# Output weights and Fourier table side by side in one tile, and products with the folded rows regrouped from 194 and 384 columns to 290 and 288

## The reference, cut to what matters

```
state = alpha[:, :, t, :, None] * state + einsum('bhd,bhe->bhde', k[:, :, t], v[:, :, t])
y[:, :, t] = einsum('bhd,bhde->bhe', q[:, :, t], state)          # stage 1: a decaying state

gate_pre = sum over 5 taps of conv_w[k] * x shifted by k         # stage 2
x = (sigmoid(gate_pre) * (x @ w_val)) @ w_out

u = x + real(fft(fft(x, axis=1), axis=2))                        # stage 3
un = (u - mean(u)) / sqrt(var(u) + 1e-06)
out = u + maximum(un @ w_ch1, 0) @ w_ch2
```

## Time and profile before

| | |
|---|---|
| median of 3 runs | 563.99 us |
| profiled execution, its own time | 564.29 us |
| its span | 562.50 us |
| PE, DVE, ACT busy | 551.8, 387.9, 215.4 us |
| granted TensorE clock | 0.995 of full speed |
| batch 1: front part (first "val" to first "h") | 182.06 to 215.53 |
| batch 1: MLP part | 215.53 to 313.49, 97.96 us |
| first "h" of batches 0, 1, 2, 3 | 82.53, 215.53, 346.96, 477.52 |

### The profile page before, as it was taken

One profiled execution on the slowest core, in us unless ns is written; L12 is line 12 of the kernel. 1 busy time (PEld: TensorE's weight loads), 2 busy tenths in 40 slices (PEclk: granted clock), 3 DMA queues, 4 the chain that ended last, 5 costly groups with the idle time before them and its releaser, 6 DMA issues.

```text
span 562.5 us, 13474 instructions
## 1 busy us (share of the span) xinstructions
PE 551.8 (98%) x5631; PEld 530.0 (94%) x5631; DVE 387.9 (69%) x870; ACT 215.4 (38%) x502; POOL 16.1 (3%) x35
## 2 busy tenths in 40 slices
PE   7999999999999999999999999999999999999995
PEld 6988999999999999999999999999999999999995
DVE  8899889978857786877676586877936474542321
ACT  5565455434352235325352135425243134222210
POOL 0010000000000000000000000000000000000000
PEclk8999999999999999999999999999999999999999
DMA  8678111332211010223111001222000000000000
GB/s 261 213 252 312 44 43 32 104 89 61 61 43 45 29 43 19 60 67 95 48 47 41 29 5 40 65 72 89 2 26 5 29 0 2 1 12 18 28 1 29
DMA packets 16235, 34.60 MB, mean 62 GB/s; under 512 B 3312, under 2 KB 6640, under 8 KB 15920
## 3 DMA queue, kind: packets, MB, share of 16 engines
q1 hardware_dynamic: 13632, 27.20, 16.0%
q0 software_dynamic: 2112, 6.29, 3.1%
q10 hardware_dynamic: 432, 0.27, 0.2%
HBM read 29.03 MB, written 4.72 MB: 60 GB/s over the span
## 4 chain that ended last, share of the span: by engine, by line
PE 94%; DVE 2%; DMA 1%; issue 1%; ACT 1%; SPq 0%; POOL 0%; DVEq 0%
PE bank L933 44%; PE bank L1018 27%; PE evens L960 4%; PE bank L1003 4%; PE bank L998 2%; PE bank L1086 2%; PE bank L1049 2%; PE sums L980 2%; PE sums L969 2%; DMA v_in<-in_v_dram 1%; PE bank L1130 1%; PE bank L1120 1%; PE bank L1055 1%; DVE w_lo L866 0%; SPq L489 0%
## 5 line engine op out<-in xcount | busy, mean ns | idle before, releaser
L915 DVE SCALAR_TENSOR_TENSOR h_lo<-bank,h_hi 128x256 fp32r<-128x256 f32 x144 | 60.5, 422 | 108.6 <-ACT h_hi L684 104.1
L933 PE MATMUL bank<-unT_hi,w_hi 128*128 128x256 f32 x432 | 124.6, 288 | 0.3 <-DVE unT_lo L691 0.2
L933 PE MATMUL bank<-unT_lo,w_hi 128*128 128x256 f32 x432 | 122.2, 283 | 0.0
L933 PE MATMUL bank<-unT_hi,w_lo 128*128 128x256 f32 x432 | 121.6, 282 | 0.0
L684 ACT ACTIVATE h_hi<-bank 128x256 fp32r<-128x256 f32 x144 | 54.8, 381 | 163.3 <-PE bank L933 163.2
L1018 PE MATMUL bank<-w_hi,h_hi 128*128 128x384 f32 x288 | 99.9, 347 | 0.0
L1018 PE MATMUL bank<-w_lo,h_hi 128*128 128x384 f32 x288 | 97.7, 339 | 0.0
L1018 PE MATMUL bank<-w_hi,h_lo 128*128 128x384 f32 x288 | 97.3, 338 | 0.0
L933 PEld LDWEIGHTS bank<-unT_hi,w_hi 128*128 128x128 f32 x432 | 81.3, 188 | 3.0 <-DVE h_lo L915 0.9
L933 PEld LDWEIGHTS bank<-unT_hi,w_lo 128*128 128x128 f32 x432 | 81.7, 189 | 0.0
L933 PEld LDWEIGHTS bank<-unT_lo,w_hi 128*128 128x128 f32 x432 | 81.5, 189 | 0.0
(11 more groups left out here) (187 smaller groups left out, 1049.5 us busy)
## 6 DMA issues: line engine op xcount, KB each, us to landing
v_in<-in_v_dram SPq DMA_DIRECT2D x24, 224.0 KB, 2.8
w_raw<-in_w_dram SPq DMA_DIRECT2D x2, 2304.0 KB, 10.7
out_dram<-u POOLq DMA_DIRECT2D x24, 192.0 KB, 2.4
a_in<-in_alpha_dram SPq DMA_DIRECT2D x44, 96.9 KB, 2.2
q_in<-in_q_dram SPq DMA_DIRECT2D x44, 96.0 KB, 2.2
k_in<-in_k_dram SPq DMA_DIRECT2D x44, 96.0 KB, 2.2
dftd<-in_dft_d_dram SPq DMA_DIRECT2D x1, 582.0 KB, 4.5
wval_raw<-in_w_val_dram SPq DMA_DIRECT2D x1, 576.0 KB, 5.2
```

The lines of the kernel that those rows point to most:

```text
L915: dve.scalar_tensor_tensor(h_lo[:, f % HBUF, :], ps[:, 0:GW], 0.0, h_hi[:, f % HBUF, :].bitcast(F32), ALU.max, ALU.subtract).then_inc(s_re ...
L933: last = pe.matmul(ps, l, r, start=(i == 0), stop=(i == len(mms) - 1))
```

## The change

The tiles wd_hi and wd_lo go. The tiles of the output weights become 772 columns wide (MIX): cosines in 0 to 193, the weights in 194 to 577, sines in 578 to 771. A product may now take any run of neighbouring columns:

- "u" takes 290: the cosines and the first 96 columns of z for the sums.
- "zsum" takes the other 288 of z.
- "v" takes 290: the last 96 columns of z for the differences, and the sines. For the first block it takes 386: the last 192 of z and the sines.
- "zdif" takes the first 288 of z for blocks 1 and 2. For the first block it is replaced by "zrow", 386 columns: the cosines and the first 192 of z.

ACT copies the z columns of each product to its place in u. The number of matmuls stays, but for "wdl", which now needs two per block of 194 columns each. All of `w_out` is needed from the first "vpre" on, where it was needed from the first "zdif" on.

```diff
+MIX = 2 * NC + D
+ZU = 96
+ZV = (192, ZU, ZU)
@@ SCHEDULE, front part
-    sch.append(("zdif", b, 0, 0))
+    sch.append(("zrow", b, 0, 0))
@@ tiles
-        WEIGHTS = [("wval", D), ("wout", D), ...
+        WEIGHTS = [("wval", D), ("wout", MIX), ...
-        wd_hi = sb("wd_hi", [128, K, 2 * NC], F32R)
-        wd_lo = sb("wd_lo", [128, K, 2 * NC], F32R)
+        mix_hi, mix_lo = w_hi["wout"], w_lo["wout"]
+        ZCOLS = slice(NC, NC + D)
+        WAVES = (slice(0, NC), slice(NC + D, MIX))
@@ loading w_out
-                            sp.dma_start(w_raw[name][:, :, :], srcs[name]).then_inc(s_wload[WN.index(name)], 16)
+                            dst = w_raw[name][:, :, ZCOLS] if name == "wout" else w_raw[name][:, :, :]
+                            sp.dma_start(dst, srcs[name]).then_inc(s_wload[WN.index(name)], 16)
@@ ACT
                 elif kind == "wd":
-                    act.activation(wd_hi[:, a, :], ps[:, 0:2 * NC], ACT.Copy).then_inc(s_hi, 1)
+                    for i, wave in enumerate(WAVES):
+                        last = act.activation(mix_hi[:, a, wave], ps[:, i * NC:(i + 1) * NC], ACT.Copy)
+                    last.then_inc(s_hi, 1)
                 elif kind == "u":
                     act.wait_ge(s_unit, done(w))
+                    act.activation(u[:, 2 * a + 1, 0:ZU], ps[:, NC:NC + ZU], ACT.Copy)
                     act.activation(U_hi[:, a, :], ps[:, 0:NC], ACT.Copy).then_inc(s_hi, 1)
                 elif kind == "vlo":
                     act.wait_ge(s_unit, done(v_))
                     if a == 0:
-                        act.activation(first_hi[0:1, :], ps[0:1, 0:NC], ACT.Copy)
-                    act.activation(V_hi[:, a, :], ps[:, NC:2 * NC], ACT.Copy).then_inc(s_hi, 1)
+                        wait_for(act, s_out, 16 * STORES * b)
+                    act.activation(u[:, 2 * a + 2, D - ZV[a]:D], ps[:, 0:ZV[a]], ACT.Copy)
+                    act.activation(V_hi[:, a, :], ps[:, ZV[a]:ZV[a] + NC], ACT.Copy).then_inc(s_hi, 1)
+                elif kind == "zrow":
+                    act.wait_ge(s_unit, done(w))
+                    act.activation(u[:, 2, 0:D - ZV[0]], ps[:, NC:NC + D - ZV[0]], ACT.Copy)
+                    act.activation(first_hi[0:1, :], ps[0:1, 0:NC], ACT.Copy).then_inc(s_hi, 1)
                 elif kind in ("zsum", "zdif"):
                     act.wait_ge(s_unit, done(w))
-                    if w[:1] + w[2:] == ("zdif", 0, 0):
-                        wait_for(act, s_out, 16 * STORES * b)
-                    act.activation(u[:, 2 * a + (1 if kind == "zsum" else 2), :], ps[:, 0:D],
-                                   ACT.Copy).then_inc(s_aread, 1)
+                    dst = u[:, 2 * a + 1, ZU:D] if kind == "zsum" else u[:, 2 * a + 2, 0:D - ZV[a]]
+                    act.activation(dst, ps[:, 0:D - ZU], ACT.Copy).then_inc(s_aread, 1)
@@ PE
                 elif kind == "wdl":
-                    pe.matmul(bank[BANK[w]][:, 0:2 * NC], neg[:, :], wd_hi[:, a, :], start=False, stop=True,
-                              skip_group_check=True).then_inc(s_unit, 1)
+                    for i, wave in enumerate(WAVES):
+                        last = pe.matmul(bank[BANK[w]][:, i * NC:(i + 1) * NC], neg[:, :], mix_hi[:, a, wave], start=False,
+                                         stop=True, skip_group_check=True)
+                    last.then_inc(s_unit, 1)
                 elif kind == "u":
-                    product(ps[:, 0:NC], [(sum_hi[:, k_, cols], sum_lo[:, k_, cols], wd_hi[:, k_, 0:NC],
-                                           wd_lo[:, k_, 0:NC]) for k_ in range(K)]).then_inc(s_unit, 1)
+                    product(ps[:, 0:NC + ZU], [(sum_hi[:, k_, cols], sum_lo[:, k_, cols], mix_hi[:, k_, 0:NC + ZU],
+                                                mix_lo[:, k_, 0:NC + ZU]) for k_ in range(K)]).then_inc(s_unit, 1)
                 elif kind in ("vpre", "v"):
-                    n = 0 if a == 0 else NC
+                    here = slice(NC + D - ZV[a], MIX)
...
+                elif kind in ("zsum", "zdif", "zrow"):
+                    here = {"zsum": slice(NC + ZU, NC + D), "zdif": slice(NC, NC + D - ZU),
+                            "zrow": slice(0, NC + D - ZV[0])}[kind]
```

More of the change, by code:

```diff
@@ L193 @@
 assert len(set(SCHEDULE)) == len(SCHEDULE)
-UNIT_KINDS = ("val", "v", "zdif", "u", "zsum", "oddrow", "pq", "pqe", "pqo", "t", "h", "out", "tapj", "wd", "wdl")
+UNIT_KINDS = ("val", "v", "zrow", "zdif", "u", "zsum", "oddrow", "pq", "pqe", "pqo", "t", "h", "out", "tapj", "wd", "wdl")
 def order_of(*kinds):
@@ L203 @@
 UNIT_AT = order_of(*UNIT_KINDS)
-HI_AT = {("v",) + w[1:] if w[0] == "vlo" else w: j for w, j in order_of("u", "vlo", "t", "h", "wd").items()}
+HI_AT = {("v",) + w[1:] if w[0] == "vlo" else w: j for w, j in order_of("u", "vlo", "zrow", "t", "h", "wd").items()}
 ACT_READ = ("zsum", "zdif", "tapj", "wdl")
 AREAD_AT = order_of(*ACT_READ)
-READS = {"pair": "pq", "vlo": "v", "comb": "pqo"}
+READS = {"pair": "pq", "vlo": "v", "zrow": "zrow", "comb": "pqo"}
 DREAD_AT = {(READS.get(w[0], w[0]),) + w[1:]: j
-            for w, j in order_of("val", "u", "vlo", "oddrow", "pair", "comb", "t", "h", "out").items()}
+            for w, j in order_of("val", "u", "vlo", "zrow", "oddrow", "pair", "comb", "t", "h", "out").items()}
 for b_ in range(B):
@@ L217, in bank_plan @@
     front_banks = {("val", 0, 0): 0, ("val", 0, 1): 3, ("val", 1, 0): 1, ("val", 1, 1): 4, ("val", 2, 0): 2, ("val", 2, 1): 0,
-                   ("v", 0, 0): 3, ("v", 1, 0): 1, ("v", 2, 0): 4, ("zdif", 0, 0): 2, ("u", 0, 0): 0, ("u", 1, 0): 3,
+                   ("v", 0, 0): 3, ("v", 1, 0): 1, ("v", 2, 0): 4, ("zrow", 0, 0): 2, ("u", 0, 0): 0, ("u", 1, 0): 3,
                    ("u", 2, 0): 1, ("zsum", 0, 0): 2, ("oddrow", 0, 0): 0, ("pq", 0, 0): 4, ("zdif", 1, 0): 3,
@@ L384, in part @@
                 return t[:, j, :]
+            if WN[i] == "wout":
+                return t[:, :, ZCOLS]
             return t[:, :, :].rearrange("p k n -> p (k n)")
@@ L592, in _ @@
                     act.wait_ge(s_unit, done(w))
-                    act.activation(wd_hi[:, a, :], ps[:, 0:2 * NC], ACT.Copy).then_inc(s_hi, 1)
+                    for i, wave in enumerate(WAVES):
+                        last = act.activation(mix_hi[:, a, wave], ps[:, i * NC:(i + 1) * NC], ACT.Copy)
+                    last.then_inc(s_hi, 1)
                 elif kind == "wdl":
                     act.wait_ge(s_unit, done(w))
-                    act.activation(wd_lo[:, a, :], ps[:, 0:2 * NC], ACT.Copy).then_inc(s_aread, 1)
+                    for i, wave in enumerate(WAVES):
+                        last = act.activation(mix_lo[:, a, wave], ps[:, i * NC:(i + 1) * NC], ACT.Copy)
+                    last.then_inc(s_aread, 1)
                 elif kind == "tapj":
@@ L892, in _ @@
                     dve.wait_ge(s_hi, hi(v_))
-                    if a == 0:
-                        dve.tensor_tensor(first_lo[0:1, :], ps[0:1, 0:NC], first_hi[0:1, :].bitcast(F32), ALU.subtract)
-                    dve.tensor_tensor(V_lo[:, a, :], ps[:, NC:2 * NC], V_hi[:, a, :].bitcast(F32),
+                    dve.tensor_tensor(V_lo[:, a, :], ps[:, ZV[a]:ZV[a] + NC], V_hi[:, a, :].bitcast(F32),
                                       ALU.subtract).then_inc(s_read, 1)
+                elif kind == "zrow":
+                    lo_part(w, first_lo[0:1, :], ps[0:1, 0:NC], first_hi[0:1, :])
                 elif kind == "oddrow":
@@ L1080, in _ @@
                         pe.wait_ge(s_flo, 2 * K * b + K - 1)
-                        pe.wait_ge(s_aread, aread(("wdl", 0, K - 1, 0)))
+                        if b == 0 and a == 0:
+                            pe.wait_ge(s_aread, aread(("wdl", 0, K - 1, 0)))
+                            weight_ready("wout")
                     else:
@@ L1084, in _ @@
                     for k_ in range(K - 1) if kind == "vpre" else (K - 1,):
-                        for x, (l, r) in enumerate(((dif_hi, wd_hi), (dif_hi, wd_lo), (dif_lo, wd_hi))):
-                            last = pe.matmul(ps[:, n:2 * NC], l[:, k_, cols], r[:, k_, n:2 * NC], start=(k_ == 0 and x == 0),
+                        for x, (l, r) in enumerate(((dif_hi, mix_hi), (dif_hi, mix_lo), (dif_lo, mix_hi))):
+                            last = pe.matmul(ps[:, 0:ZV[a] + NC], l[:, k_, cols], r[:, k_, here], start=(k_ == 0 and x == 0),
                                              stop=(k_ == K - 1 and x == 2))
@@ L1089, in _ @@
                         last.then_inc(s_unit, 1)
-                elif kind in ("zsum", "zdif"):
-                    if b == 0 and kind == "zdif" and a == 0:
-                        weight_ready("wout")
+                elif kind in ("zsum", "zdif", "zrow"):
                     high, lo = (sum_hi, sum_lo) if kind == "zsum" else (dif_hi, dif_lo)
-                    product(ps[:, 0:D], [(high[:, k_, cols], lo[:, k_, cols], w_hi["wout"][:, k_, :],
```

(5 more changed lines are left out.)

3 lines of the change are left out of this document (2 added, 1 removed).

## The result

Over 22 runs of each kernel, the changed one takes 566.78 us (median), the one before 564.74. The ratio is 1.0029, with a 95% interval of 1.0017 to 1.0041: slower, by about 1.6 us (1.0 to 2.3). (The ratio is that of the means, 566.45 and 564.81; the medians lie 2.0 apart.) I had forecast 564.6, which is +0.6 us over the 563.99 of the kernel before and too little to be told from no change. The direction was the one I had argued for, the size was not.

What follows compares the result with a forecast made beforehand. PE was 98% busy, but with thin slack over a DVE chain unbroken in batches 1 and 2. Terms +0.67 + 0.40 + 0.40 - 0.83 + 0.05 = +0.69 us on 563.99 gave 564.68, hence 564.6; 8-in-10 range 563.0 to 565.8.

Steps and rivals of the forecast that it cites:

- Nothing outside it changes: Outside each batch's front part (first "val" to first "h"), nothing changes except a few prologue products; val and MLP 0.
- The oddrow wait: PE before "oddrow", after U_lo of the last "u": 0.08 of 0.60 us slack left, so nothing counted.
- PE's column costs: PE matmuls, line between 256 and 384 columns: 290 cost 0.1334 us, 288 cost 0.1326; PE alone -0.83 us per batch.
- a rule for a warm matmul: PE starts every N / 2.4 GHz plus 2.5 ns, so regrouping gives PE nothing; as rival 567.5 or so, chance 0.01.
- The copy ahead of U_hi: ACT's 96-column copy in each "u" holds U_hi for 0.15 us (0 to 0.33), on the path.
- The rival that it holds ACT for its full time: "u" stage, all four batches: narrow copy holds ACT 0.30 to 0.33 us instead of 0.15; 565.3, chance 0.20.
- Batches 1 and 2: U_lo 2 comes 1.17 us later, DVE's run has no gap, PE waits before the transposes: +0.40 each.
- Batch 0: Front part: U_lo 2 late by 0.99 us, DVE's idle 0.32 before oddsum absorbs some: +0.67.
- Batch 3: Front part without attention work on DVE: "h" starts at 476.69 instead of 477.52, -0.83 us.
- 0.08 off the whole: Pipelining guesses judged more likely too slow than too fast, so 564.68 became 564.6.
- the milder rival: ACT and DVE catch up half the charge in batches 0 to 2 (0.7), batch 3 gives 1.24: 563.2, chance 0.09.

Runs made afterwards that it cites:

- experiment 1: Kernel before, plus 128 unused bytes per partition below all the weights, shifting x, folded rows, unT and h; ratio 0.9993.
- experiments 2 and 9: 2: changed kernel plus 384 unused bytes below the weights, 1.0001. 9: kernel before plus 128 unused bytes below u, above the h and unT regions, 0.9993.
- Experiment 7: Changed kernel, with ACT's copy of the 96 z columns of each "u" placed after U_hi and U_lo instead of ahead of U_hi; ratio 1.0020.
- experiment 5: Changed kernel, with DVE's second scan moved behind "oddrow" and its scaling behind "inverse" in batches 1 and 2; ratio 0.9996.
- the differences half: Changed kernel with only "v" and "zdif" regrouped, "u" back at 194 and "zsum" at 384, no narrow copy; ratio 0.9973 to the kernel before.
- the sums half: Changed kernel with only "u" and "zsum" regrouped, "v" of blocks 1 and 2 at 194 and "zdif" at 384; ratio 1.0023 to the kernel before.
- the same move: DVE's second scan behind "oddrow", scaling behind "inverse", batches 1 and 2: on the kernel before 1.0007, on the changed kernel 0.9996.
- experiments 8 and 11: One kernel twice: changed, only differences regrouped, 384 unused bytes, DVE's second scan and scaling moved in batches 1 and 2; 0.9969, then 0.9961 in more rounds.

## Why the prediction was wrong, step by step

- **"Nothing outside it changes": the step that failed.** The prediction's first paragraph left val and the MLP out of the sum, since neither their code nor their operands change. Their operands' addresses do, and what stands ahead of the first "h" does. The val products cost +0.39 in all, and experiments 1 and 2 show that it is their place in SBUF. The MLP parts and the last stretch are longer by 0.27 altogether. Of this 0.22 is one matmul in each of batches 1, 2 and 3: the first "h" product, which now has waited for unT_lo, takes 0.19 to 0.20 to the next start (218.07 to 218.26) where it took 0.12 to 0.13. In batch 0 it had waited before too, and there the part grew by 0.02 only. The other 0.05 I could not assign.
- **The oddrow wait: counted as nothing, costs 0.14 to 0.16** in every batch. My text had 0.08 of slack left and took that for what a semaphore needs. "oddrow" starts 0.14 behind the end of U_lo (205.52 to 205.66), which is 0.07 later than zsum 0 would have let it, and then its own first step is 0.08 longer. Experiment 7 removes both. In batches 1 and 2 this stop is not on the chain that ends last.
- **PE's column costs: right.** The line between 256 and 384 gave 0.1334 for 290; 27 "u" took 3.63 to 3.69 us, 0.134 to 0.137 each. Nine zsum 0 products took 1.28 with the stop behind them and 1.21 without it (experiment 7), against 1.19 by the line. The Trainium skill, "TensorE: Matmul & The Clock Gate", section "Wait — 56ns, not 53.3ns?", has a rule for a warm matmul by which the regrouping moves no time on PE. The trace disagrees: 194 and 384 columns cost 284 ns together, 290 and 288 cost 268, and with the stop removed (experiment 5) v to h fell below that of before.
- **The copy ahead of U_hi: right** (0.15 taken, 0.14 measured). The rival that it holds ACT for its full time falls with that row.
- **Batches 1 and 2: right in mechanism, +0.40 forecast, +0.49 measured.** The last U_lo came 1.20 later after the first "v" product (1.17 forecast), and unT_lo ended where I had it, 24.42 us after that product. What I had too small was the last step: "h" starts 0.15 behind that end, where I had 0.09.
- **Batch 0: +0.67 forecast, +0.47 measured.** "u" began 0.12 later, where I had 0.23, so the last U_lo was late by 0.85 and not 0.99. DVE's idle time then took up 0.39, where I had 0.32.
- **Batch 3: -0.83 forecast, -0.64 measured.** From zdif 1 to "h" it gave 1.03 of the 1.07 that I had. The rest is all ahead of it: the first "v" to zdif 1 grew by 0.39 where I had 0.24, and that is the stop at "oddrow".
- Together: fronts +0.16 over the forecast, val +0.39, MLP and end +0.27, in all +0.82, which takes +0.64 to +1.46. I had also taken 0.08 off the whole because my steps seemed too slow; for the fronts together they were too fast.
- **The time itself missed 564.6 by 2.2 us, and 0.75 of it is no mechanism.** The three runs I had of the kernel before gave 563.99, and the 22 runs give 564.74: the reference was too low by chance. Moved up by that, the range would end at 566.55, still below 566.78. Another 0.4 is that the changed kernel's median lies 0.33 above its mean and that of before 0.07 below. One sum of the prediction was off as well: the milder rival comes to 563.5 by its own terms, not 563.2.

## What to carry to other kernels

Widening a product to spare another helps only where the time that it frees lies on the chain that ends last: find out which products stand ahead of the run on the other engine and which behind it, and widen as little as can be ahead of it. Here both halves shortened what stands behind by the same 0.74 per batch in the forecast, but the differences half delayed the other engine's run by 0.43 in batch 1 and the sums half by 0.79. The first was worth 0.3%. The second, better by the engine's own count, lost 0.2%. Then give the second engine room at the same time; the same move that was worth nothing before (24.09) was worth 0.8 us per batch after. And a tile that changes its size moves all the tiles below it: keep their offsets, or measure an untouched stage.

## What the runs showed of the hardware that was not expected

The pace of the val products and of the MLP part depends on where the two operands of a matmul start in SBUF, relative to each other. From the sizes of the tiles, the distance of w_val from x, modulo 256 bytes, is 0 in the kernel before and in experiments 2 and 9 (54 products of 384 columns in 9.36 to 9.38 us) and 128 in the changed kernel and experiment 1 (9.50 to 9.51): 1.4%. The distance of w1 from unT is 128 in the kernel before and the changed one (MLP part 97.94 to 98.02) and 0 in experiments 1, 2 and 9 (97.54 to 97.64): 0.4%. The distance of w2 from h is the same as that of w1 from unT in all five. All five placements fit this one statement. For the val products alone the place of x would do as well, since w_val never moves. It is the MLP part that needs the distance: modulo 256, unT stands alike in the changed kernel (slow) and in experiments 1 and 9 (fast), and w1 stands alike in the kernel before (slow) and in experiments 1 and 9 (fast). It was tried at these two distances only, was not looked at for the short groups of products with the folded rows, and what in the chip makes it is open. Groups of the by-line view of the kernel before and of experiment 1 show it for both kinds of the MLP's products, in their mean durations:

```profile
L933 PE MATMUL bank<-unT_lo,w_hi 128*128 128x256 f32 x432 | 122.2, 283 | 0.0
...
L1018 PE MATMUL bank<-w_lo,h_hi 128*128 128x384 f32 x288 | 97.7, 339 | 0.0
```

```profile
L934 PE MATMUL bank<-unT_lo,w_hi 128*128 128x256 f32 x432 | 121.6, 281 | 0.0
...
L1019 PE MATMUL bank<-w_lo,h_hi 128*128 128x384 f32 x288 | 96.7, 336 | 0.0
```

The second: the prologue of one and the same kernel took 1.6 us more in one profile than in the other, together with a lower clock granted in its first 20 us (0.91 and 0.83, experiments 8 and 11). All 13 profiles fit: the first "val" starts at 48.86 to 49.68 in the six with 0.91, at 50.19 to 51.32 in the six with 0.83, and at 51.92 in the one with 0.74. That is as much as the whole effect of this change, and the reason why many runs were needed to see it.
